# Attention scores in unsplit fp32 on the two row halves of the array, for two batches at once, in a fused attention and mixture-of-experts kernel

## The reference

```
q, k, v: (4 batches, 8 heads, 576, 64) fp32
scores = (q @ k.T) / 8
thresh = max(scores, -1) - tau                 # tau = 0.02
attn   = exp(where(scores >= thresh, scores, -1e9) - max)
attn   = attn / (sum(attn, -1) + 1e-9)
x      = (attn @ v) as 2304 tokens x 512
x      = top-1 mixture of 8 experts(x)         # 512 -> 1024 -> 512, relu, gated
out    = sum over 4 experts of p[e] * (relu(x @ w1[e]) @ w2[e])
```

## Time and profile before

| what | us |
|---|---|
| median of three runs | 1516.47 |
| lowest, highest | 1514.25, 1516.54 |
| the profiled execution | 1516.2 |
| its span, first to last instruction | 1514.4 |
| PE busy (share) | 1460.5 (96%) |
| DVE busy (share) | 792.5 (52%) |
| ACT busy (share) | 642.1 (42%) |

### The profile page before, as it was taken

One profiled execution on the slowest core, in us unless ns is written; L12 is line 12 of the kernel. 1 busy time (PEld: TensorE's weight loads), 2 busy tenths in 40 slices (PEclk: granted clock), 3 DMA queues, 4 the chain that ended last, 5 costly groups with the idle time before them and its releaser, 6 DMA issues.

```text
span 1514.4 us, 27992 instructions
## 1 busy us (share of the span) xinstructions
PE 1460.5 (96%) x10480; PEld 1303.5 (86%) x10480; DVE 792.5 (52%) x1310; ACT 642.1 (42%) x1328; POOL 149.3 (10%) x274
## 2 busy tenths in 40 slices
PE   7999999998399999999999999999999999999999
PEld 6888888886388888889999999999989999999998
DVE  6888888886767777776322233222252222432222
ACT  6888888884256666664222222111131111311111
POOL 2111111110111112211000000000000000000000
PEclk9999999999599999999999999999999999999999
DMA  5444444441568888886200002000030000100001
GB/s 117 95 104 105 98 109 101 99 102 33 176 224 281 280 278 281 294 289 233 85 1 1 0 21 91 1 1 1 1 112 1 0 1 0 57 21 22 22 21 42
DMA packets 169702, 143.94 MB, mean 95 GB/s; under 512 B 96256, under 2 KB 140384, under 8 KB 169632
## 3 DMA queue, kind: packets, MB, share of 16 engines
q1 hardware_dynamic: 160560, 120.37, 27.4%
q0 software_dynamic: 6640, 21.97, 4.1%
q10 hardware_dynamic: 2432, 0.59, 0.2%
HBM read 111.56 MB, written 16.12 MB: 84 GB/s over the span
## 4 chain that ended last, share of the span: by engine, by line
PE 80%; DVE 11%; issue 5%; ACT 2%; DMA 2%; SPq 0%; DVEq 0%; POOL 0%; ACTq 0%; POOLq 0%
PE S L729 11%; PE S L731 11%; PE S L730 11%; PE bank L742 8%; PE bank L744 8%; PE bank L743 8%; DVE pr L1012 3%; PE S L624 3%; PE S L743 3%; PE S L744 3%; PE S L742 3%; PE S L588 3%; PE bank L637 2%; DVE qb L981 2%; DVE nmax L1026 2%
## 5 line engine op out<-in xcount | busy, mean ns | idle before, releaser
L892 ACT ACTIVATE hth<-S 128x384 fp32r<-128x384 f32 (+1 forms) x264 | 121.6, 462 | 675.5 <-PE S L731 673.2
L729 PE MATMUL S<-xch,wh 128*128 128x384 f32 (+1 forms) x1056 | 339.5, 322 | 4.3 <-DVE xcl L1206 4.1
L731 PE MATMUL S<-xch,wl 128*128 128x384 f32 (+1 forms) x1056 | 339.1, 321 | 0.0
L730 PE MATMUL S<-xcl,wh 128*128 128x384 f32 (+1 forms) x1056 | 339.0, 321 | 0.0
L1212 DVE SCALAR_TENSOR_TENSOR htl<-S,hth 128x384 fp32r<-128x384 f32 (+1 forms) x264 | 136.7, 520 | 289.3 <-ACT hth L892 286.6
L742 PE MATMUL bank<-wh,hth 128*128 128x512 f32 x584 | 229.4, 393 | 2.5 <-DVE htl L1226 2.5
L744 PE MATMUL bank<-wh,htl 128*128 128x512 f32 x584 | 227.7, 390 | 0.0
L743 PE MATMUL bank<-wl,hth 128*128 128x512 f32 x584 | 227.6, 390 | 0.0
L1198 DVE TENSOR_TENSOR wl<-ring,wh 128x1024 fp32r<-128x1024 f32 x160 | 191.4, 1222 | 56.4 <-ACT wh L883 52.1
L729 PEld LDWEIGHTS S<-xch,wh 128*128 128x128 f32 x1056 | 200.3, 190 | 6.8 <-DVE xcl L1206 4.5
L730 PEld LDWEIGHTS S<-xcl,wh 128*128 128x128 f32 x1056 | 200.3, 190 | 1.2
(11 more groups left out here) (204 smaller groups left out, 1851.6 us busy)
## 6 DMA issues: line engine op xcount, KB each, us to landing
ring<-in_moe_w SPq DMA_DIRECT2D x160, 512.0 KB
raw<-in_k SPq DMA_DIRECT2D x36, 128.0 KB, 2.4
tokens_x<-x_nat SPq DMA_DIRECT2D x16, 288.0 KB, 5.0
x_nat<-compact_y POOLq DMA_DIRECT2D x6, 768.0 KB, 6.9
raw<-in_q SPq DMA_DIRECT2D x34, 128.0 KB, 3.1
vv<-in_v SPq DMA_DIRECT2D x34, 128.0 KB, 2.3
qb<-qa SPq DMA_DIRECT2D x16, 224.0 KB, 3.2
qa<-qb SPq DMA_DIRECT2D x16, 224.0 KB, 3.5
```

The costliest lines, as they stand in the source:

```text
L729: pe.matmul(hb(f, n), w1_block(wh, kk, f), xch[:, kk, 0:n], start=kk == 0, stop=False)
L730: pe.matmul(hb(f, n), w1_block(wh, kk, f), xcl[:, kk, 0:n], start=False, stop=False)
L731: last = pe.matmul(hb(f, n), w1_block(wl, kk, f), xch[:, kk, 0:n], start=False, stop=kk == KD - 1)
```

## The change

Only the attention is rewritten. Queries and keys stay in plain fp32 (`qt`, `kt`): batch one of the pair on partitions 0 to 63, batch two on 64 to 127. There is no split, no `qb`, `kl`, and no swap by SP. A unit is now five steps (`STEPS`): four pairs of tiles, one tile of each batch, and one step (`FULL`, i = 4) for the last 64 rows of the first batch and the first 64 of the second. Scores of a pair are four unsplit fp32 matmuls, of 448 and 128 columns for each batch; batch one uses the upper 64 rows of the array and `S0`, batch two the lower 64 rows and `S1` or `S2` in turn (`near`). Because `S0` serves every pair, PE waits before the scores for the previous pair's first mask. The probabilities of a pair (1152 columns) are turned in nine blocks. Outputs of a pair are copied in one instruction, with a lag of three steps, and the turns of the next unit's q and k come all at once in the step `FULL`, those of their 64-row tails in the step i = 0. POOL normalizes in thirds.

```diff
-            def step(h, j, zero_h, values_only=False, turn=True):
-                ...
-                            ops = [(a[bp][:, s * P:(s + 1) * P], kt[bp][:, k0 + n * HK:k0 + (n + 1) * HK])
-                                   for s, k0 in parts for a in (qa, qb)]
-                            for i, (a, b) in enumerate(ops):
-                                last = pe.matmul(S[j % 3][:, n, 0:HK], a, b, start=i == 0, stop=i == len(ops) - 1)
+            def values(j, to):
+                ...
+                    groups = [(0, (first, first)), (1, (second, second))]
+                for c, halves in groups:
+                    for n in range(5):
+                        for half in range(2):
+                            ...
+                            last = pe.matmul(ob(to, c, lo, lo + HALF), pt[j % 2][:, p, lo:lo + HALF], vv[bp][:, v, :],
+                                             start=n == 0, stop=n == 4)
+            def scores(j):
+                ...
+                f, g = scored(j, 0), near(j)
+                if i == FULL:
+                    q0, q1 = a[lo, 4 * P:SEQ], a[hi, 0:HALF]
+                    pe.matmul(f[lo, OFF:512], q0, b[lo, 0:FB], start=True, stop=True)
+                    pe.matmul(f[hi, OFF:512], q1, b[hi, TAIL:TAIL + FB], start=True, stop=True)
+                    pe.matmul(f[lo, 512:512 + P], q0, b[lo, FB:SEQ], start=True, stop=True)
+                    pe.matmul(f[hi, 512:512 + HALF], q1, b[hi, TAIL + FB:SEQ], start=True, stop=True)
+                    pe.matmul(f[hi, 512 + HALF:512 + P], q1, b[hi, 0:TAIL], start=True, stop=True).then_inc(s_scores, 1)
+                    return
+                q0, q1 = a[lo, i * P:(i + 1) * P], a[hi, HALF + i * P:HALF + (i + 1) * P]
+                pe.matmul(f[:, OFF:512], q0, b[lo, 0:FB], start=True, stop=True)
+                pe.matmul(g[:, OFF:512], q1, b[hi, 0:FB], start=True, stop=True)
+                pe.matmul(f[:, 512:512 + P], q0, b[lo, FB:SEQ], start=True, stop=True).then_inc(s_scores, 1)
+                pe.matmul(g[:, 512:512 + P], q1, b[hi, FB:SEQ], start=True, stop=True).then_inc(s_scores, 1)
+            def step(h, j, zero_h, last=False):
+                ...
+                if i == 0:
+                    pe.wait_ge(s_qd, u + 1)
+                    pe.wait_ge(s_kd, u + 1)
+                    pe.wait_ge(s_td, u + 1)
+                if i != FULL and not (zero_h and j < 1):
+                    pe.wait_ge(s_prob, done - 1 if i > 0 else done)
+                scores(j)
+                if i == FULL and not last_unit(last, bp):
+                    pe.wait_ge(s_raw[1 - bp], 96 * (h + 1))
+                    pe.wait_ge(s_prob, done - 1)
+                    prep(S[0][:, 0, :], 1 - bp, QR).then_inc(s_tq, 1)
+                    prep(S[0][:, 1, :], 1 - bp, KR).then_inc(s_tk, 1)
+                if not (zero_h and j < 1):
+                    pe.wait_ge(s_prob, done)
+                    if not (zero_h and j < 2):
+                        pe.wait_ge(s_evac, n - 1)
+                    ...
+                    turn((j - 1) % US, near(j + 1))
+                if i == 0 and not last_unit(last, bp):
+                    pe.wait_ge(s_rt[1 - bp], 64 * (h + 1))
+                    prep(TX, 1 - bp, TR, 1).then_inc(s_tt, 1)
+                if not (zero_h and j < 2):
+                    ...
+                    pe.wait_ge(s_evac, n - 1)
+                    pe.wait_ge(s_blk, n - 1)
+                    values((j - 2) % US, near(j + 1)).then_inc(s_val, 1)
...
# ACT, step
+                act.wait_ge(s_scores, done + tiles_in(j))
+                if not (zero_h and j < 2):
+                    pair_blocks((j - 2) % US, near(j))        # one 128x128 copy into pt
+                if not (zero_h and j < 3):
+                    outputs(h if j >= 3 else h - 1, (j - 3) % US, near(j))   # one copy of 2 x 65
+                for t in range(tiles_in(j)):
+                    act.wait_ge(s_nmax, done + t + 1)
+                    ...
+                    act.activation(ex[(x + t) % 2][:], sc(j, t), ACT.Exp, bias=nmax[:, x + t:x + t + 1]).then_inc(s_exp, 1)
+                if i == FULL and not (last and bp == 1):
+                    act.wait_ge(s_tq, 2 * h + bp + 2)
+                    queries(1 - bp, S[0][:, 0, :])            # one 128x512 activation into qt
+                if not (zero_h and j < 1):
+                    act.wait_ge(s_turned, n)
+                    evacuate((j - 1) % US).then_inc(s_evac, 1)   # two 128x512 copies
...
# DVE, step
+                for t in range(tiles_in(j)):
+                    dve.wait_ge(s_scores, done + t + 1)
+                    if t == tiles_in(j) - 1 and not (zero_h and j < 2):
+                        ...
+                            dve.wait_ge(s_ov, n - 2)
+                    dve.tensor_reduce(nmax[:, x + t:x + t + 1], sc(j, t), AX.X, ALU.max, negate=True).then_inc(s_nmax, 1)
+                if i == FULL and not (last and bp == 1):
+                    dve.wait_ge(s_tk, 2 * h + bp + 2)
+                    dve.tensor_copy(kt[1 - bp][:, 0:4 * P], S[0][:, 1, :]).then_inc(s_kd, 1)
+                for t in range(tiles_in(j)):
+                    dve.wait_ge(s_exp, done + t + 1)
+                    dve.wait_ge(s_thr, done + t + 1)
+                    ...
+                    dve.scalar_tensor_tensor(pr[j % 2][:, t * SEQ:(t + 1) * SEQ], sc(j, t), thr[:, x + t:x + t + 1],
+                                             ex[(x + t) % 2][:], ALU.is_ge, ALU.mult).then_inc(s_prob, 1)
...
# SP, start of the program: tau comes after six loads instead of four
-            load_start(sp, slice(0, DH), tau_too=True)
+            load_q(sp, 0, 0, s_q0)
+            load_tail(sp, 0, 0, s_t0)
+            sp.dma_start(tau1[:], tau.rearrange("(a b) -> a b", a=1).to_broadcast([P, 1])).then_inc(s_tau, 16)
# POOL: 3 normalizations of 3 tiles per unit, after the thresholds 6, 7 and 8 of the next unit
+                    if at_x in (6, 7, 8) and not (first and bp == 0):
+                        normalize(h if bp == 1 else h - 1, 1 - bp, at_x - 6)
```

More of the change, by code:

```diff
@@ L511, in _ @@
                 head(h, False)
-            normalize(HEADS - 1, 1)
+            for part in range(3):
+                normalize(HEADS - 1, 1, part)
             def gather(m, b):
@@ L640, in _, with prep @@
-            for j in range(UT):
+            def prep(to, bp, first, n=4):
+                for t in range(n):
+                    last = pe.transpose(to[:, t * P:(t + 1) * P], raw[bp][:, first + t, :], ident[:])
+                return last
+            pe.wait_ge(s_cst, 2)
+            pe.wait_ge(s_q0, 32)
+            prep(TP, 0, QR).then_inc(s_tq, 1)
+            pe.wait_ge(s_t0, 64)
+            prep(S[2][:, 0, :], 0, TR, 1).then_inc(s_tt, 1)
+            pe.wait_ge(s_k0, 64)
+            prep(TX, 0, KR).then_inc(s_tk, 1)
@@ new lines, in turn, with last_unit @@
+            def turn(j, to):
+                buf = pr[j % 2]
+                for kb in range(4):
+                    pe.transpose(TP[:, kb * P:(kb + 1) * P], buf[:, kb * P:(kb + 1) * P], ident[:])
+                if tiles_in(j) == 2:
+                    for kb in range(4):
+                        pe.transpose(TX[:, kb * P:(kb + 1) * P], buf[:, (5 + kb) * P:(6 + kb) * P], ident[:])
+                pe.transpose(blk(to), buf[:, 4 * P:5 * P], ident[:]).then_inc(s_turned, 1)
+            def last_unit(last, bp):
+                return last and bp == 1
@@ L641, in _ @@
+            for j in range(US):
                 step(0, j, True)
-            with pe.Fori(1, HEADS) as h:
-                for j in range(UT):
+            with pe.Fori(1, HEADS - 1) as h:
+                for j in range(US):
                     step(h, j, False)
-            for j in range(LAG_V):
-                step(HEADS, j, False, values_only=True, turn=j < LAG_T)
-            pe.wait_ge(s_ov, UT * HEADS)
-            pe.wait_ge(s_evac, UT * HEADS)
+            for j in range(US):
+                step(HEADS - 1, j, False, True)
@@ L651, in _ @@
+            pe.wait_ge(s_evac, US * HEADS - 1)
+            pe.wait_ge(s_blk, US * HEADS - 1)
+            values(US - 2, flat(S[0])).then_inc(s_val, 1)
+            pe.wait_ge(s_prob, UT * HEADS)
+            turn(US - 1, near(US + 1))
+            pe.wait_ge(s_evac, US * HEADS)
+            pe.wait_ge(s_blk, US * HEADS)
+            pe.wait_ge(s_ov, US * HEADS - 2)
+            values(US - 1, near(US)).then_inc(s_val, 1)
+            pe.wait_ge(s_ov, US * HEADS)
             pe.wait_ge(s_bc, 19)
@@ L862, in _, with pair_blocks, outputs @@
-            for j in range(UT):
+            act.wait_ge(s_tq, 1)
+            queries(0, TP[:])
+            act.wait_ge(s_tt, 1)
+            tails(0, S[2][:, 0, 0:P])
+            def pair_blocks(j, src):
+                act.copy(pt[j % 2][:, 4, :], blk(src)).then_inc(s_blk, 1)
+            def outputs(h, j, src):
+                bp, i, _ = at(j)
+                if i == 0 and not (isinstance(h, int) and h == 0):
```

(16 more changed lines are left out.)

412 lines of the change are left out of this document (164 added, 248 removed).

## The result

The changed kernel takes 1491.26 us (median of 4, 1489.40 to 1493.05) where the kernel before takes 1516.26: a ratio of 0.984 [0.982, 0.986]. The profiled execution took 1492.81 with a span of 1491.0. The forecast was 1491.0.

The account below looks back on a forecast made before the run. Three nearly full engines bound attention; after the change, the S0 loop bounds pairs and PE bounds FULL. Last values 24.8 us sooner plus 0.5 from normalization: 1516.2 - 25.3 = 1490.9, on the median's footing 1491; range 1474 to 1518.

Parts of the forecast that it names:

- PE's own pair: PE's work for a pair of tiles: scores 1.27, nine turns 1.08, values 1.30, sum 3.65 us against 4.65 before.
- the switch from row halves to the whole array: On PE between a pair's scores and its turns: cost taken as 0.20 us, bounds 0 and 0.40.
- over 0.3 the hand-overs are dearer: Sign: PE should wait about 0.1 us for the mask before a pair's scores; over 0.3 means dearer hand-overs.
- The loop: First tile's scores, reduce, exp, mask, back to PE through S0: 3.75 us a pair, 0.10 over PE's own 3.65.
- `FULL`: Step from the fourth pair's first reduce to the next unit's: 8.18 us, decided by PE, which waits for nothing.
- The unit: Attention unit of four pairs and FULL: 3 x 3.75 + 8.18 = 19.43 us against 20.93 before.
- Start and end: Attention's ends: first scores at 8.85, half clock adds 2.5, drain 7.2, last values at 324.9 instead of 349.7 us.
- Row halves in turn: Rival: pair scores on the two row halves stream one after another, 1.92 instead of 0.96; 1563 us; chance 0.12.
- Overlap in part: Rival: the row halves' score streams overlap only partly or run slower; about 1514 us, range 1500 to 1516; chance 0.16.
- `FULL` serialized by its bank: Rival: FULL's two halves writing one bank run in turn, 0.9 more on PE, 14 us in all, 1505; chance 0.08.
- Clock: Rival: PE's clock falls in attention, some 15 us for a unit at half clock; chance 0.06, shared with other stalls.
- Cheaper hand-overs: Rival: loop below PE's 3.65, a pair gains 0.10, 1486 us; 1478 with free switches in FULL; no separate chance.

Follow-up runs that it names:

- e2: The changed kernel with the value products of three of five key blocks left out, the loop's work kept: 1479.22 us, ratio 0.976.
- e3: The changed kernel with the exp of each pair's first tile covering 288 of 576 columns from the second head on: 1481.64 us, ratio 0.978.
- r0: The changed kernel run again unaltered, on another chip, in five rounds: 1489.74 us, ratio 0.983 to the kernel before.
- e1: The changed kernel with each pair's second tile reading batch one's partitions, so both tiles use one row half; FULL unchanged: 1547.87 us, ratio 1.021.
- e5: The changed kernel with 12 unused identity turns on PE before the queries land and 6 before the first scores: 1489.38 us, ratio 0.983.
- e7: The changed kernel with scores cut at 322 columns, first tile's exp and mask in two parts, tau and k earlier, 12 and 5 idle turns: 1484.34 us, ratio 0.979.

## Why the prediction was right

*PE's own pair:* 3.65 forecast, 3.62 measured for the fourth pair. Within it the switch from row halves to the whole array, bounded 0 to 0.40 and taken as 0.20, took 0.10: the last records of the scores start at 199.89, the turns at 200.10, where a record of this size holds the array for 0.11 (199.78 to 199.89). What the prediction had wrong is that every pair has this work. It gave nine turns and the values of two tiles to each, but `FULL` has one tile, so pair 1 has 3.3 and pair 2 has 3.1. PE's idle time is therefore not 0.10 in each pair but 0.4 to 0.7 in two and 0.1 in the third. The time didn't suffer from it, since the loop decides in just these steps; but the sign "over 0.3 the hand-overs are dearer" would have misled, as a wait this long comes from PE's smaller load.

*The loop:* forecast 3.75 (its terms add up to 3.74), measured 3.80 in most steps. To the first reduce 1.28 (forecast 1.28), reduce to exp 0.79 (0.79), mask and hand-over to PE as forecast. The mis-sized term is the hand-over from exp to mask. Exp takes 0.74 and not 0.77, and the mask starts 0.12 after its end (200.99 to 201.85 is 0.86), where I took 0.04. But 0.12 is not the price of this pair of engines. In the last unit, from the timeline of the kernel after:

```profile
317.49 1.41 ACT L911 ACTIVATE ex<-S,nmax 128x576 f32<-128x576 f32 x2 [0.31 <-DVE nmax L1072]
...
318.27 1.54 DVE L1081 SCALAR_TENSOR_TENSOR pr<-S,thr,ex 128x576 f32<-128x576 f32 x2
```

Here it is 0.78, so 0.04 after the exp's end, as forecast. It is 0.77 or 0.78 in 13 of 15 steps of the units written out (the first unit apart); in the looped heads it is 0.86 (once 0.92), but for the second pair of every second unit (0.78). In the same units the step from reduce to exp, too, is 0.87 instead of 0.79 in the first pair (208.31 to 209.18). The instructions are the same in both parts; in the loop the numbers that the waits compare with are worked out from the loop's variable. That this adds the 0.08 is my best guess, and no run tests it. e2 shows that the loop over `S0` decides (PE's work away, nothing gained), e3 that it does so down to PE's own work, which only the third pair step reached.

*`FULL`:* 8.18 forecast, 8.11 measured in the step shown, 8.08 by the medians; PE goes through it without a wait, as the walk said. The unit: 19.43 forecast, 19.48 measured. The right sum hid an incomplete view: the walk saw PE as the limit of the step out of `FULL` and the short copies as that of the step into it. e2 moved the step into `FULL` by 0.54 through PE's work alone (the short copies wait for PE's scores of `FULL`), so PE is the limit behind both.

*Start and end:* `tau` used at 7.12 (7.4), first scores 8.50 (8.85), the cold start 3.8 (2.5), of which 1.0 lies before the first reduce and 2.8 in the first unit (in r0 1.0 and 1.4), drain 7.57 (7.2), last values 326.62 (324.9). The 1.7 late are these terms: 1.3 for the cold start, 0.5 for the next 14 units and 0.1 less in the last, in all 1.65 between first and last scores, 0.37 of drain, less 0.35 at the start. The 0.5 for normalizations in thirds can't be told within the 2.5 by which the tail scatters. By the profiled executions the change gave 23.4 of the 25.3 forecast; by the medians 25.0. That the forecast fell within 0.3 of the median is luck to that extent.

*The rivals.* Row halves in turn: refuted by e1, which shows the price too. It came out at 1548 and not 1563; e1 leaves `FULL` on its diagonal, and the prediction had 0.9 a unit there, 14 us. Overlap in part: the records start 0.01 apart, and the second tile's stream costs nothing. The Trainium skill ("TensorE: Matmul & The Clock Gate", "Measured speedup vs the span model") gives 3.07 for four row tiles; two tiles of 64 rows lost nothing here, so its ratio doesn't carry over to them. `FULL` serialized by its bank: L612 and L613 write the same banks on different partitions from different row halves and start 0.01 apart, twice. The rule of the Trainium skill ("TensorEngine Tiling (Array Packing)", "Gotcha 1: PSUM Pressure"), by which different row tiles don't use one bank at a time, doesn't show in this trace; the measurement decides. Clock: 1.00 in the window. Cheaper hand-overs: in the looped heads the one from exp to mask was dearer, in those written out it was as forecast.

## What to carry to other kernels

When three engines are nearly full, walk the loop that a buffer closes, hand-over by hand-over, and compare it with the bottleneck's own work in each step separately: here 3.8 against 3.3, 3.1 and 3.6, and an experiment on either limit moves only the steps where it decides. Take a hand-over from a row of the same two engines in the same part of the program, since one pair of instructions had 0.12 in the looped heads and 0.04 in those written out. Before you read a small gain at the start from one profile, see how far the cold start varies by itself: here 1.9 us.

## What was unexpected of the hardware

- The second tile's first record starts 0.01 after the first tile's first and 0.47 ahead of the first tile's second, though both records of the first tile's matmul stand ahead of it in the program. With both tiles on one half (e1) the first tile's two records come first. So the two halves don't keep one common order of starts.
- Two 64 by 64 tiles on a diagonal, writing the same banks on different partitions, run side by side: 0.43 and 0.38 a record, 0.01 apart.
- The hand-over from ACT's exp to DVE's mask costs 0.12 in most steps of the looped heads and 0.04 in the heads written out, with the same instructions; the cause is open.
- With the same program the first unit took 20.37 to 22.25 us, and PE's records got short at 17.0 to 22.3 us. With the clock already at 2.4 GHz it fell again after a wait of 2.24 us (e5); with waits of 1.79 and 1.30 it stayed up (e7).
